# Moving one batch of gate logits across the last attention pair of a linear-attention and mixture-of-experts kernel

## The reference, cut to what matters

```python
# q, k, v, f_logit: (4, 8, 768, 48)
f = 1 / (1 + exp(-f_logit))
for t in range(S):
    state = f[t, :, None] * state + outer(k[t], v[t])
    y[t] = q[t] @ state
x = y.transpose(0, 2, 1, 3).reshape(3072, 384)
# first mixture
logits = normalise(x) @ normalise(expert_emb).T / tau      # 8 experts
expert = argmax(logits); gate = softmax(logits)[expert]
out = gate * (relu(x @ w1[expert]) @ w2[expert])
# second mixture: the same with its own weights on the rows whose x @ w_skip > 0, plus x
```

## Time and profile before

| | |
|---|---|
| time, median of 3 runs | 695.41 us (694.36 to 696.84) |
| the profiled execution's own time | 694.36 us |
| its span, first to last instruction | 692.6 us |
| TensorE busy | 650.4 us, 94% of the span |
| VectorE, ScalarE, GpSimd busy | 434.2, 305.8, 171.6 us |
| mean granted TensorE clock | 0.970 of 2.4 GHz |
| attention | from the start to 182 us |
| first expert matmul | 212.6 us |

### The profile page before, as it was taken

The page is one execution under the profiler, slowest core; times in us unless marked ns, Lnnn a source line. Parts: engine busy times, 40 slices in busy tenths (PEclk is TensorE's granted clock), DMA queues, the critical chain, the costliest instruction groups (busy, mean ns, idle before and its releaser), DMA issues.

```text
span 692.6 us, 15660 instructions
## 1 busy us (share of the span) xinstructions
PE 650.4 (94%) x5042; PEld 622.4 (90%) x5043; DVE 434.2 (63%) x931; ACT 305.8 (44%) x514; POOL 171.6 (25%) x195
## 2 busy tenths in 40 slices
PE   5999999999839999999999999997699999999997
PEld 4999999999839999999999999996699999999997
DVE  5888988979636563838182937564276546557652
ACT  3665666656304343534242533332156336436640
POOL 5321244262430004041304133132301110110111
PEclk9999999999759999999999999999799999999999
DMA  9385886662144261707071727341385374474610
GB/s 187 73 165 123 194 188 145 127 167 59 70 134 163 98 225 60 256 33 267 23 251 35 256 69 242 100 148 40 95 283 178 145 262 128 148 237 142 238 38 23
DMA packets 144217, 100.68 MB, mean 145 GB/s; under 512 B 106319, under 2 KB 135098, under 8 KB 144176
## 3 DMA queue, kind: packets, MB, share of 16 engines
q1 hardware_dynamic: 137008, 87.42, 43.9%
q0 software_dynamic: 7168, 12.73, 5.1%
HBM read 79.46 MB, written 30.08 MB: 158 GB/s over the span
## 4 chain that ended last, share of the span: by engine, by line
PE 89%; issue 4%; DVE 3%; ACT 2%; DMA 1%; DVEq 0%; SPq 0%; POOL 0%; POOLq 0%
PE bank_a L948 8%; PE bank_a L950 7%; PE bank_a L949 7%; PE banks_y L818 6%; PE banks_s L797 4%; PE banks_y L957 4%; PE banks_y L959 3%; PE banks_y L958 3%; PE banks_y L971 3%; PE banks_y L810 3%; PE bank_b L948 2%; PE bank_b L949 2%; PE bank_b L950 2%; PE banks_y L749 2%; PE bank_b L957 2%
## 5 line engine op out<-in xcount | busy, mean ns | idle before, releaser
L1368 DVE TENSOR_TENSOR w_lo<-raw_w,w_hi 128x768 fp32r<-128x768 f32 x128 | 115.0, 951 | 45.6 <-ACT w_hi L1104 45.6
L1104 ACT ACTIVATE w_hi<-raw_w 128x768 fp32r<-128x768 f32 x128 | 99.1, 835 | 10.4 <-issue 10.4
L948 PE MATMUL bank_a<-x_hi,w_hi 128*128 128x384 f32 (+2 forms) x288 | 98.4, 342 | 3.5 <-issue 1.5
L950 PE MATMUL bank_a<-x_hi,w_lo 128*128 128x384 f32 (+2 forms) x288 | 95.4, 331 | 0.0
L949 PE MATMUL bank_a<-x_lo,w_hi 128*128 128x384 f32 (+2 forms) x288 | 95.4, 331 | 0.0
L648 POOL DMA_INDIRECT sorted_rows<-row_send,slot_idx x32 | 34.0, 1063 | 212.7 <-DVE slot_idx L1696 205.4
L658 POOL DMA_INDIRECT out<-row_send,out_idx x24 | 24.8, 1032 | 173.5 <-DVE row_send L1763 160.6
L948 PEld LDWEIGHTS bank_a<-x_hi,w_hi 128*128 128x128 f32 x288 | 54.1, 188 | 9.0 <-issue 5.3
L950 PEld LDWEIGHTS bank_a<-x_hi,w_lo 128*128 128x128 f32 x288 | 54.1, 188 | 0.8
L949 PEld LDWEIGHTS bank_a<-x_lo,w_hi 128*128 128x128 f32 x288 | 54.2, 188 | 0.7
L1291 ACT ACTIVATE h_hi<-bank_a 128x384 fp32r<-128x384 f32 (+1 forms) x48 | 21.6, 450 | 74.1 <-PE bank_a L950 74.0
(11 more groups left out here) (269 smaller groups left out, 1565.8 us busy)
## 6 DMA issues: line engine op xcount, KB each, us to landing
raw_w<-in_moe_w SPq DMA_DIRECT2D x30, 1536.0 KB
sorted_rows<-pad_row SPq DMA_DIRECT2D x8, 582.0 KB
raw_f<-in_f_logit SPq DMA_DIRECT2D x32, 144.0 KB, 3.1
raw_k<-in_k SPq DMA_DIRECT2D x32, 144.0 KB, 3.2
raw_q<-in_q SPq DMA_DIRECT2D x32, 144.0 KB, 3.6
raw_v<-in_v SPq DMA_DIRECT2D x32, 144.0 KB, 2.9
xs<-sorted_rows SPq DMA_DIRECT2D x11, 388.0 KB, 3.3
xs<-sorted_rows SPq DMA_DIRECT2D x19, 194.0 KB, 3.0
```

The source lines that it names most:

```text
L948: pe.matmul(bank, hi, x_hi[:, kd, 0:size], start=(kd == 0), stop=False)
L950: ins = pe.matmul(bank, lo, x_hi[:, kd, 0:size], start=False, stop=(kd == KD - 1))
L1104: act.activation(w_hi[:, sl, :], raw_w[:, sl, :], ACT.Copy).then_inc(w_split_hi, 1)
L1368: dve.tensor_tensor(w_lo[:, sl, :], raw_w[:, sl, :], w_hi[:, sl, :].bitcast(F32), ALU.subtract).then_inc(w_split_lo, 1)
```

## The change

`logits(KD * B - 2, ps_logit_end)`, the logits of part 10, is issued on TensorE directly after the safety count's matmul in the head of pair 15, no more at the end of the pair's tail. TensorE's wait for `safe_known`, which stood ahead of it, moves behind pair 15, ahead of the logits of part 11. VectorE's `add_logits` for part 10 moves from behind the four weight slices to a place ahead of the copy of the safety count.

```diff
@@ TensorE, pair_head, last pair
                 else:
                     pe.wait_ge(safe_ready, 1)
                     pe.matmul(ps_safe, safe_b[:], ones[:, 0:1], start=True, stop=True).then_inc(safe_summed, 1)
+                    logits(KD * B - 2, ps_logit_end)
@@ TensorE, pair_tail
                 from_scores(par, 1).then_inc(y_ready, 1)
-                if last:
-                    pe.wait_ge(safe_known, 1)
-                    logits(KD * B - 2, ps_logit_end)
@@ TensorE, after the pairs
             transpose_x(KD * B - 1)
             pe.wait_ge(gs[0]["logit_read"], KD * B - 1)
+            pe.wait_ge(safe_known, 1)
             logits(KD * B - 1, ps_logit_end)
@@ VectorE, pair_tail
                 if not last:
                     scale_q(ch, g + 1, 1 - par)
                 else:
+                    add_logits(ch, KD * B - 2, ps_logit_end)
                     dve.wait_ge(safe_summed, 1)
                     dve.tensor_copy(safe_count[:], ps_safe).then_inc(safe_known, 1)
                     place_tokens(ch, rows[b % 3])
@@
                 if last:
                     for sl in range(SLICES // 2):
                         split_lo(0, sl)
-                    add_logits(ch, KD * B - 2, ps_logit_end)
```

## The result

The changed kernel took 703.42 us (median of 13 runs, 698.95 to 706.37) against 695.41 us of the kernel before (692.93 to 700.63). The ratio of the two on the same chips is 1.0087, with a 95% interval of 1.0065 to 1.0108: 4.5 to 7.5 us slower. Two later comparisons of the same pair gave 1.0072 (1.0045 to 1.0099) and 1.0084 (1.0050 to 1.0117). I take +5 to +6 us as the thing to explain; that the first median lies 8 us up is more than any of the ratios, and the surplus of some 2 us isn't explained here. The forecast was +2.8 us.

The account below looks back on a forecast made before the run. The prediction took TensorE's chain of waits around the last attention pair as the bound. It summed -1.75 + 2.2 + 1.9 + 0.4 = +2.75, say +2.8 us, to 698.2 on the median, range 697.4 to 699.9.

Parts of the forecast that it names:

- the wider range: Range of whole-kernel time, leaving out the third rival and the tip of the second: 694.9 to 701.2 us.
- the clock under pair 15: Clock falls at 181.0 us, so nearly all 24 records of pair 15's part from the scores run at 1.2 GHz: +1.9 us.
- Logits leave the old place: After pair 15, part 11's transposes wait 0.74 us for the copy of y instead of 2.49 of logits: -1.75 us.
- Logits arrive: In pair 15's head, 0.8 us pause for x_t plus 1.34 us of logits at 2.4 GHz delay the second score half: +2.2.
- The bound above: Clock falls once the moved logits are through, at 178.7, stretching pair 15's first two groups too: an estimated +2.1 us more.
- Second rival: Clock falls at once behind the moved logits: +4.9 to +5.7 us, 700.3 to 701.1; chance 0.23.
- VectorE, GpSimd, SyncE at 0: Later work on these engines is covered by existing waits: cost 0; without cover at most 0.2 on VectorE, 0.1 on the others.
- The warm-up: The 60 matmuls starting at 204.88, shifted later, may meet the clock's return later: 0 to 1.2 us, taken as +0.4.
- Third rival: Clock holds through part 11 and VectorE's norm path decides its sum: -1.7 us, 693.7; chance 0.10.
- the price of the move at an unchanged clock: The moved logits' late arrival less the gain at their old place, with no clock effect: 2.2 - 1.75 = +0.45 us.

Follow-up runs that it names:

- after_again: The changed kernel run once more with nothing edited; ratio to the kernel before 1.0072 (1.0045 to 1.0099).
- after_third: The changed kernel again, unedited, on the chip of the last three runs; ratio to the kernel before 1.0084 (1.0050 to 1.0117).
- fill: The changed kernel with 12 unused matmuls in the pause ahead of part 10's logits; ratio to the kernel before 1.0033 (1.0011 to 1.0055).
- pause: The kernel before plus a TensorE wait for part 10's x_t ahead of pair 15's second score half; ratio 1.0031 (0.9999 to 1.0062).
- place: The changed kernel with part 10's logits issued behind pair 15's second score half; ratio to the kernel before 1.0019 (0.9995 to 1.0042).
- wide_after: fill with the logits of parts 10 and 11 made 64 columns wide; ratio to the kernel before 1.0021 (0.9998 to 1.0043).
- wide_before: The kernel before with parts 10 and 11 logits 64 columns wide, 6 and 18 unused matmuls added; ratio 0.9979, run again 1.0009.
- pause_filled: pause with 12 unused matmuls ahead of its added wait; ratio to the kernel before 1.0002 (0.9965 to 1.0039).

## Why the prediction was wrong

The sign was right, and so was the kind of loss; the size wasn't. The forecast was +2.8 us, in a range of its own of +2.0 to +4.5; the ratios say +5 to +6, and the median of 703.42 us is past the upper end of the wider range too. The step that failed is the term for the clock under pair 15, sized at 1.9 us. I had taken the fall of the one profiled execution, 181.0, as a moment that the move could only bring forward, and then left it where it was, so that L818 alone was slow. In the three profiles of the changed kernel it came at 177.1, 177.5 and 179.1, and the term is 3.54 us in one and 4.8 in the others.

- *Logits leave the old place:* forecast -1.75, measured -2.49 + 0.72 = -1.77. Right. The transposes cost 0.16 more, since the first no longer runs beside the last record of the logits.
- *Logits arrive:* forecast +2.2, measured 2.15 to the next group when they run at the upper level. Right. In after_again they ran at 1.2 GHz and took 2.73 us, 1.2 more than the 1.50 in the profile of the kernel after. I had taken the upper level for them because the one profile that I had showed no fall ahead of 181.
- *The clock under pair 15:* forecast 1.9. Measured in the profile of the kernel after: 0.69 (second score half) + 0.74 (from the state) + 2.11 (from the scores) = 3.54; in after_again and after_third also the logits, 1.23. Their stretch of 18.64 is 5.3 over before. The price of one record at the lower level, 0.10 us, was right: L818 and its like take 2.82 us in fill and 5.30 here, 0.10 for each of the 24 records. What the kernel before paid already was 0.37 of it (3.19 against 2.82), not 0.5. What was wrong is how many instructions stand behind the fall. The bound above, "as soon as the logits are through", wasn't one either: in two profiles the fall came ahead of the logits or as they began (0.8 and 1.0 after L784; they start about 0.96 after it).
- *Second rival* (fall right behind the logits, +4.9 to +5.7 with the warm-up, chance 0.23): nearest to what happened. What I held against it, that part 9's logits hadn't brought the clock down, compared them with a place where no pause stood ahead. What makes the fall early stays open: pause and place have one as early without the moved logits, place even without a pause. Shown is that it was early in all three profiles of the changed kernel, and that the mean clock of its timed runs is lower (0.966 and 0.964 against 0.969 and 0.967).
- *VectorE, GpSimd, SyncE at 0:* right while the clock falls. VectorE's sum of part 11 still waits for L749, 1.23 us in both profiles (and 1.23 after), GpSimd's sends ended before the next ones. With the clock held it's no more right: wide_after ends on VectorE's slices.
- *The warm-up:* forecast +0.4. From part 11's sum to the first expert matmul: 23.05 in the kernel after, 23.51 in after_again, 23.45 in after_third, against 23.04: 0 to 0.5. Right. One reading ahead of it wasn't quite: the warm-up of the second mixture didn't run wholly at 1.2 GHz, its last 0.4 us ran at 2.4. The sum doesn't use this.
- *Third rival* (clock holds, -1.7): wide_after made it hold. VectorE ended last as I had it, with a stretch of 12.12 us where I had 11.5, so 1.2 us of the stretch were gained. The kernel was still 1.5 us slower by its ratio, and this difference isn't accounted for. In the changed kernel itself the clock fell in all three profiles.

5.3 of stretch and 0.5 of warm-up make the +5 to +6 us of the ratios. With one execution profiled at a time I can't say how the falls are distributed over the timed runs; three of three profiles of the changed kernel had it 0.8 to 2.4 us after L784, and the one of the kernel before 4.7. It may come earlier in other executions of that kernel, as place suggests. Also open is a part that the profiles don't place: fill's profile is back at the old stretch, and its ratio is at +2.3 us. And the price of the move at an unchanged clock, +0.45 in the forecast, is 0.7 to 1.3 us by the stretches of wide_after against the two of wide_before, since VectorE ends last there.

The Trainium skill, "TensorE: Matmul & The Clock Gate", section "HAM oscillation", names waits of TensorE as what brings the clock down. I had weighed that against a fall at full busy share and set it aside. The runs lean its way for the pause (mean clock 0.965 against 0.969 with it, 0.970 against 0.967 with it filled; pause 2.2 us slower, pause_filled 0.1, with overlapping intervals), though this pause of 0.7 us is far shorter than those of the page. The traces of before and place disagree with it as the only cause, as their falls had no pause ahead. By the rule read on its own the kernel would have kept its clock.

## What to carry to other kernels

A clock fall that one profile shows at a given moment isn't a fact of that moment. It came 4.7 us after L784 in the kernel before, 0.8 to 2.4 in the changed one, and 0.2 in a kernel that had run the same work up to there as the kernel before. All matmul work behind it took 1.8 to 1.9 times as long. So take several profiles before a forecast leans on such a moment. When matmul work is moved to a place where it must wait for its input, price everything behind the wait at the lower clock as a likely case, and try whether unused matmuls in the pause take some of it back (here 2.3 us in place of 5 to 6). And once the clock is held, read again which engine ends last.

## What the runs showed of the hardware

- The granted clock of one kernel fell at 177.1, 177.5 and 179.1 us in three executions, with L784 at 176.06, 176.74 and 176.75. The stretch from L784 to part 11's sum differed by 1.2 us between them without any edit.
- The clock fell with TensorE busy 1.00 of the windows ahead of it: in before at 181.0, and in place at 178.0, before anything that place had changed had run.
- Fp32 matmuls of 128x128 weights took 0.11 us a record at 2.4 GHz and 0.21 to 0.23 at 1.2 GHz with 8 columns; with 64 columns 0.12 at 2.4 GHz (1.43 us for 12).
- 12 unused bf16 matmuls of 128 columns took 0.78 us at 2.4 GHz. Put into a wait of about 0.7 us they made it 0.1 us longer.
